# Attention's opening: the second pair's stack half written, half sent, and the first head's score rows in four banks

## The reference

```python
scores = scale * np.matmul(q, k.transpose(0, 1, 3, 2))        # [B, H, 576, 576]
scores = np.where(causal, -1000000000.0, scores)
a = np.exp(scores - scores.max(-1, keepdims=True))
a /= a.sum(-1, keepdims=True) + 1e-09
local = np.matmul(a, v)
q_p = phi(q)                                                   # elu(q) + 1
mem_out = einsum('bhsd,bhde->bhse', q_p, M_prev) / (einsum('bhsd,bhd->bhs', q_p, z_prev)[..., None] + 1e-06)
g = 1 / (1 + exp(-beta))
x = g * mem_out + (1 - g) * local
```

## Time and profile before

| what | value |
|---|---|
| median of 3 runs | 820.97 us |
| the profiled execution | 821.17 us, of which its span 819.4 us |
| TensorE busy | 810.7 us, 99% of the span |
| DVE, ACT, POOL busy | 510.4, 339.6, 339.1 us |
| granted TensorE clock, mean | 0.999 |
| transfers | 49.45 MB |

### The profile page before, as it was taken

How to read it: one execution, slowest core, us unless ns; L and a number is a source line. 1 busy time by engine, 2 the same in 40 slices (tenths; PEclk the granted TensorE clock), 3 DMA queues, 4 the chain that set the end, 5 groups by cost and what they waited for, 6 DMA issues and landing times.

```text
span 819.4 us, 14574 instructions
## 1 busy us (share of the span) xinstructions
PE 810.7 (99%) x5630; PEld 704.2 (86%) x5630; DVE 510.4 (62%) x1052; ACT 339.6 (41%) x608; POOL 339.1 (41%) x453
## 2 busy tenths in 40 slices
PE   8999999999999999999999999999999999999998
PEld 7788888888888888888888899999998888888886
DVE  7877777776588653333433353346688977777762
ACT  6766776675422232222322232233436434333431
POOL 6667676676899930000000000005268844443300
PEclk9999999999999999999999999999999999999999
DMA  8587777866134320000000000000111000000001
GB/s 152 128 178 154 173 167 155 178 142 144 53 103 116 95 73 1 1 1 0 1 1 0 1 1 1 1 1 1 52 51 52 26 27 26 26 14 27 26 14 51
DMA packets 86371, 49.45 MB, mean 60 GB/s; under 512 B 65056, under 2 KB 73248, under 8 KB 86304
## 3 DMA queue, kind: packets, MB, share of 16 engines
q1 hardware_dynamic: 83760, 47.94, 24.3%
q10 hardware_dynamic: 2544, 0.59, 0.4%
HBM read 27.28 MB, written 4.72 MB: 39 GB/s over the span
## 4 chain that ended last, share of the span: by engine, by line
PE 96%; DVE 1%; issue 0%; ACT 0%; POOL 0%; POOLq 0%
PE ps_h L1297 8%; PE ps_y L1313 8%; PE ps_h L1298 8%; PE ps_h L1299 8%; PE ps_y L1314 8%; PE ps_y L1312 8%; PE ps_v L678 5%; PE ps_s L591 4%; PE ps_r L1766 4%; PE ps_r L1764 4%; PE ps_r L1765 4%; PE ps_hid L1701 4%; PE ps_hid L1699 4%; PE ps_hid L1700 3%; PE ps_x L657 3%; PE ps_x L658 3%
## 5 line engine op out<-in xcount | busy, mean ns | idle before, releaser
L1414 DVE TENSOR_TENSOR xT<-xT 128x512 f32<-128x512 f32 (+1 forms) x80 | 61.2, 765 | 127.7 <-ACT xT L1372 127.7
L1598 POOL TENSOR_TENSOR win<-stage,win 128x512 fp32r<-128x512 f32 x2 | 2.6, 1296 | 282.4 <-ACT win L1833 282.4
L1314 PE MATMUL ps_y<-g_hi,wout 128*128 128x512 f32 (+1 forms) x320 | 117.5, 367 | 0.0
L1313 PE MATMUL ps_y<-g_lo,wout 128*128 128x512 f32 (+1 forms) x320 | 117.5, 367 | 0.0
L1312 PE MATMUL ps_y<-g_hi,wout 128*128 128x512 f32 (+1 forms) x320 | 117.4, 367 | 0.0
L1378 ACT ACTIVATE g_hi<-xT 128x512 fp32r<-128x512 f32 (+1 forms) x80 | 47.3, 591 | 135.0 <-DVE xT L1416 135.0
L1297 PE MATMUL ps_h<-x_hi,win 128*128 128x512 f32 (+1 forms) x280 | 103.0, 368 | 0.0
L1299 PE MATMUL ps_h<-x_hi,win 128*128 128x512 f32 (+1 forms) x280 | 102.8, 367 | 0.0
L1298 PE MATMUL ps_h<-x_lo,win 128*128 128x512 f32 (+1 forms) x280 | 102.8, 367 | 0.0
L1372 ACT ACTIVATE xT<-ps_h 128x512 f32<-128x512 f32 (+1 forms) x80 | 44.3, 554 | 139.0 <-PE ps_h L1299 137.2
L1419 DVE TENSOR_TENSOR g_lo<-xT,g_hi 128x512 fp32r<-128x512 f32 (+1 forms) x80 | 65.1, 813 | 52.6 <-ACT g_hi L1378 52.6
(11 more groups left out here) (220 smaller groups left out, 1814.6 us busy)
## 6 DMA issues: line engine op xcount, KB each, us to landing
stacked<-cut SPq DMA_DIRECT2D x56, 288.0 KB, 4.8
out<-res SPq DMA_DIRECT2D x18, 256.0 KB, 2.0
v_raw<-in_v SPq DMA_DIRECT2D x32, 128.0 KB, 2.7
stage<-in_moe_w_in SPq DMA_DIRECT2D x16, 256.0 KB, 2.8
stage<-in_moe_w_out SPq DMA_DIRECT2D x16, 256.0 KB, 2.7
k_raw<-in_k SPq DMA_DIRECT2D x28, 128.0 KB, 2.6
q_raw<-in_q SPq DMA_DIRECT2D x28, 128.0 KB, 3.6
stage<-in_moe_w_in SPq DMA_DIRECT2D x4, 512.0 KB, 3.5
```

What stands on the lines that cost most here:

```text
L1313: pe.matmul(out, wout[:, f, HI, w], g_lo[:, r, 0:n], start=False, stop=False)
L1314: ins = pe.matmul(out, wout[:, f, LO, w], g_hi[:, r, 0:n], start=False, stop=(f == FT - 1))
L1414: dve.tensor_tensor(r, r, r, ALU.mult).then_inc(square_done, 1)
```

## The change

- `DIRECT` goes from 2 to 1: only pair 0 is written in place. Pair 1 is cut like the later ones, but only half of its stack is sent: SP's new `stack(1)` issues two DMAs of 288 KB instead of four, for the halves on the partitions where the parts don't lie already, and ACT writes the other halves with two copies out of `cut` (`third_head`, `fourth_head`: 64 partitions by 2 x 576). SP's order becomes: part of pair 0, keys 1, queries 1, keys 2, queries 2, stack(1), values 0, memory, keys 3, queries 3, values 1, stack(2), keys 4 and on as before.
- Pair 0's six loads are shared: SP issues the first head's key tiles, the half tiles of the keys and the second head's query tiles; ACT the rest. The second pair's loads are all SP's.
- Head 0's score rows: rows 3, 0 and 2 go into the two banks of `ps_x` (`X_AT`), so that TensorE writes all five rows without waiting for a maximum.
- TensorE's order: the second pair's exchanged turns go (ten transposes), its plain turns come after head 0's third rows, head 1's first rows come before head 0's maxima are turned; `WARM` is 8, and two of the `keep_warm` groups go while one changes its place and size.
- POOL: the two doublings go, `repeat_first` for pair 1 goes, `low_queries` is now the first pair's and comes before the first `spread_maxima`, and one memset of 1.5 us comes after it (`fill_others`). ACT: six of the second pair's copies become `round_second_queries`, `round_keys(1)` and the two copies named above; `repeat_queries(1, ...)` is new (two copies). DVE: `low_second_queries` and `cut_keys(1)` take the place of the second pair's four low parts, and `work_out_rest` is moved from after `second_rows(3)` to before `first_rows(2)`.

```diff
 
...
+    DIRECT = 1
+    BY_ACT = ["k_own0", "k_moved0", "q_hi0", "q_cut0", "q_hi1", "q_own1", "third_head", "fourth_head"]
+    BY_DVE = ["k_own1", "k_moved1", "q_lo0"]
+    K_SWAPPED, Q_SWAPPED = 1, 2
...
-    WARM, WARM_BETWEEN = 10, 5
+    WARM, WARM_BETWEEN = 8, 5
...
+    def stack_landed_at(p):
+
+        return 16 * (STACK_DMAS * stacks_sent(p) - (1 if p % SLOTS == 1 else 0))
...
     def cut_is_free(eng, p):
         if p >= DIRECT + 2:
             stacks_taken(eng, p - 2)
-        else:
-            dve_placed(eng, p - 2, "q_lo0")
-
...
+            if p == 3:
+                act_placed(eng, "fourth_head")
+        elif p == 2:
+            dve_placed(eng, "q_lo0")
...
+    def score_rows(h, t):
+
+        if h == 0 and t in X_AT:
+            bank, at = X_AT[t]
+            return ps_x[:, bank, at:at + keys[t]]
+        return ps_s[:, S_AT[t]:S_AT[t] + keys[t]]
...
@@ -304,15 +318,21 @@
             for par in range(2):
                 arrived = stack_landed[p % SLOTS][par]
                 mine, to = words(cut[p % 2][MINE[par], :, :]), slot(2 * p + par)
-                sp.dma_start(words(stacked[0:D, to, :, 0:S]), mine[:, Q_HI:K_HI + 1:2, :]).then_inc(arrived, 16)
-                sp.dma_start(words(stacked[D:P, to, :, 0:S]), mine[:, Q_LO:K_HI + 1, :]).then_inc(arrived, 16)
-
-        load_keys(0)
+                if p > 1 or par == 1:
+                    sp.dma_start(words(stacked[0:D, to, :, 0:S]), mine[:, Q_HI:K_HI + 1:2, :]).then_inc(arrived, 16)
+                if p > 1 or par == 0:
+                    sp.dma_start(words(stacked[D:P, to, :, 0:S]), mine[:, Q_LO:K_HI + 1, :]).then_inc(arrived, 16)
+
+        whole_tiles(sp, first_k, k, 0, 0, k_in[0])
+        half_tiles(sp, first_k, k, 0, k_in[0])
+        whole_tiles(sp, first_q, q, 0, 1, q_in[0])
         load_keys(1)
+        tiles(sp, q_raw[1], q, 1, q_in[1])
         load_keys(2)
         load_queries(2)
+        stack(1)
+        load_values(0)
         load_memory()
-        load_values(0)
         load_keys(3)
         load_queries(3)
         load_values(1)
...
+            pool.wait_ge(cleared, POOL_CLEARS - 1)
+
+        def fill_others():
             pool.memset(words(K1[MINE[0], 1:LATE, 1, 0:S]), 1.0).then_inc(cleared, 1)
             pool.wait_ge(cleared, POOL_CLEARS)
...
+        def repeat_first():
+            act_placed(pool, "q_hi0")
+            pool.tensor_scalar(Q1[MINE[0], 0, 0, 0:S], words(stacked[MINE[0], slot(0), 0, 0:S]), 1.0, 1.0,
                                ALU.mult, ALU.mult).then_inc(repeated, 1)
...
+            act_placed(pool, "q_own1")
+            pool.wait_ge(qT_copied, 1)
+            pool.tensor_tensor(stacked[MINE[1], slot(1), 0, 0:S], qT[0][MINE[1], :], Q1[MINE[1], 0, 1, 0:S],
                                ALU.subtract).then_inc(low_by_pool, 1)
...
-        double(first_k[1], k_in[1])
-        double(first_q[1], q_in[1])
-        pool.wait_ge(doubled_pool, 2)
-        repeat_first(0)
+        repeat_first()
         pool.wait_ge(repeated, 1)
         clear_others()
-        repeat_first(1)
-        pool.wait_ge(repeated, DIRECT)
-        spread_maxima(0)
         low_queries()
         pool.wait_ge(low_by_pool, 1)
+        spread_maxima(0)
+        fill_others()
...
             elif p == 1:
-                act_placed(pe, 0, "k_own0")
+                pe.wait_ge(cleared_dve, DVE_CLEARS + 1)
+                act_placed(pe, "k_own0")
                 pe.wait_ge(k_lo_done, 1)
...
+            rows = score_rows(h, t)
...
+        def turn_maxima(h):
+            need(pe, maxed, 4 * (h + 1))
+            return pe.transpose(ps_s[:, NEG_AT:NEG_AT + P], least[h % 2][:, :], ident[:, :])
...
         def first_rows(h):
             if h == 0:
                 pe.wait_ge(cleared, FOR_ROWS)
...
+                act_placed(pe, "q_hi1")
+                dve_placed(pe, "q_lo0")
+            elif h == 1:
+                act_placed(pe, "q_own1")
+                pe.wait_ge(low_by_pool, 1)
+                pe.wait_ge(maxed, 2)
             elif h < HEADS:
                 p = h // 2
-                pe.wait_ge(stack_landed[p % SLOTS][h % 2], 16 * STACK_DMAS * stacks_sent(p))
-            need(pe, maxed, 4 * min(h, HEADS))
-            if is_head(h - 1):
-                ins = pe.transpose(ps_s[:, NEG_AT:NEG_AT + P], least[(h - 1) % 2][:, :], ident[:, :])
+                pe.wait_ge(stack_landed[p % SLOTS][h % 2], stack_landed_at(p))
+                if p == 1:
+                    act_placed(pe, ("third_head", "fourth_head")[h % 2])
+            if is_head(h - 1) and h != 1:
+                ins = turn_maxima(h - 1)
             if h < HEADS:
                 rows_of_scores(h, 4)
                 ins = rows_of_scores(h, 1)
-            ins.then_inc(scored, 1)
+            if h != 1:
+                ins.then_inc(scored, 1)
...
         def second_rows(h):
-            pe.wait_ge(maxed, 4 * h + 1)
+            need(pe, maxed, 4 * h + 1 if h > 0 else 0)
             rows_of_scores(h, 3).then_inc(scored, 1)
 
         def third_rows(h):
-            pe.wait_ge(maxed, 4 * h + 2)
+            need(pe, maxed, 4 * h + 2 if h > 0 else 0)
             need(pe, neg_done, h)
             rows_of_scores(h, 0)
             rows_of_scores(h, 2).then_inc(scored, 1)
...
             a, p, par = slot(h), h // 2, h % 2
             kept = KEPT[par]
             if h == 0 and c == 0:
-                pe.wait_ge(k_lo_done, 1)
-                act_placed(pe, 1, "q_hi1")
-                dve_placed(pe, 1, "q_lo0")
+                pe.wait_ge(maxed, 4)
                 pe.wait_ge(cleared, FOR_FIRST)
...
             if c == 0:
                 pe.wait_ge(neg_spread, h + 1)
                 if p < DIRECT:
-                    pe.wait_ge(repeated, p + 1)
-                    act_placed(pe, p, "q_own1")
-                    pe.wait_ge(k_lo_done, p + 1)
+                    pe.wait_ge(repeated, 1)
+                    act_placed(pe, "q_own1")
                 else:
...
                 need(pe, t_loc_done, p)
                 if h < 2:
-                    act_placed(pe, 1, "k_own1")
+                    pe.wait_ge(k_hi_done, 1)
                     pe.wait_ge(k_lo_done, 2)
...
         warm_up()
         turn_keys(0)
-        turn_swapped_keys(0)
+        turn_swapped_keys()
         turn_queries(0)
-        turn_swapped_queries(0)
-        act_placed(pe, 0, "k_moved0")
-        dve_placed(pe, 0, "k_moved1")
+        turn_swapped_queries()
+        act_placed(pe, "k_moved0")
+        dve_placed(pe, "k_moved1")
         keep_warm(ps_x[:, 0, 0:P])
         first_rows(0)
-        turn_swapped_keys(1)
-        pe.wait_ge(qT_copied, 1)
-        keep_warm(ps_t[:, 0:P])
         second_rows(0)
+        third_rows(0)
+        turn_queries(1)
         turn_keys(1)
-        turn_queries(1)
-        third_rows(0)
-        turn_swapped_queries(1)
-
         first_rows(1)
-        act_placed(pe, 1, "q_hi1")
-        keep_warm(ps_x[MINE[0], 0, 0:P], 4)
+        turn_maxima(0).then_inc(scored, 1)
+        keep_warm(ps_x[:, 0, 0:P])
+
         cross(0, 0)
         second_rows(1)
         cross(0, 1)
@@ -809,8 +813,9 @@
...
     def scalar(act):
-        tiles(act, first_q[0], q, 0, q_in[0])
-        tiles(act, first_q[1], q, 1, q_in[1])
+        whole_tiles(act, first_k, k, 0, 1, k_in[0])
+        whole_tiles(act, first_q, q, 0, 0, q_in[0])
+        half_tiles(act, first_q, q, 0, q_in[0])
         act.dma_start(beta_in[:, :], beta.unsqueeze(0).broadcast_to([P, H])).then_inc(beta_landed, 16)
...
+            elif what in ("third_head", "fourth_head"):
+                act.wait_ge(k_hi_done, 1)
+                act.wait_ge((q_hi_done, q_lo_done)[what == "fourth_head"], 1)
+                own, to = ((Q_HI, 2), (Q_LO, 3))[what == "fourth_head"]
+                half = MINE[to - 2]
+                place, source = stacked[half, to, :, 0:S], words(cut[1][half, own:K_HI + 1:K_HI - own, :])
...
-        for p, what in BY_ACT:
-            put(p, what)
-            if what == "q_own1":
-                copy_queries(p)
-                if p == 0:
-                    open_gates()
+        def round_second_queries():
+            act.wait_ge(qT_turned, 2)
+            act.activation(cut[1][:, Q_HI, :], ps_t[:, 0:S], ACT.Copy).then_inc(q_hi_done, 1)
+
+        for what in BY_ACT[:-2]:
+            put(what)
+        copy_queries(0)
+        open_gates()
+        round_second_queries()
+        copy_queries(1)
+        round_keys(1)
+        put("third_head")
         exp_weights(0, 0)
         feature_relu(0)
         exp_weights(0, 1)
@@ -903,12 +920,15 @@
         exp_weights(0, 2)
         feature_exp(0)
         exp_weights(0, 3)
+        put("fourth_head")
         round_keys(2)
 
         exp_weights(1, 0)
         feature_relu(1)
         exp_weights(1, 1)
         feature_exp(1)
+        repeat_queries(1, 0)
+        repeat_queries(1, 1)
         exp_weights(1, 2)
         repeat_queries(2, 0)
         exp_weights(1, 3)
...
-            if h == 1:
```

(62 more changed lines are left out.)

120 lines of the change are left out of this document (40 added, 80 removed).

## The result

The changed kernel takes 822.92 us in the median of 12 runs (822.21 to 824.65), the kernel before 821.33 beside it on the same chip (820.72 to 821.90). The ratio is 1.0020, 95% interval 1.0012 to 1.0028. The forecast was 820.8 with a range up to 822.7, so the result lies outside it, on the slow side. The profiled execution took 823.08 us, its span 821.3 [before: 819.4].

The account below looks back on a forecast made before the run. TensorE's lateness in the opening was taken to bound the kernel; the opening's 1.3 us gain, handed back at heads 4 and 6 by the transfer queue, left -0.15: 820.97 - 0.15 = 820.8 us, range 819.0 to 822.7.

Parts of the forecast that it names:

- `z_prev`'s last: Memory loads on SP: issued from about 17.7, the last landing at 24.5, half a microsecond before it is needed.
- the sum for `stack(2)`: SP's queue: half stack at 14.15, two issues 1.3, sixteen loads 12.3, giving 27.8; 27.6 taken, ends 26.5 and 29.1.
- Rival (c): Memory part: z_prev lands at 25.5 instead of 24.5, memory at 25.6, total 820.4; chance 0.07.
- Rival (b): SP's queue binds hard: stack(2) at 29.1, head 6's half 1.35 late, total 822.3, up to 823; chance 0.20.
- The slip: SP's queue: stack(2) 0.6 us late, stack(3) likewise; ends at stack(4), where SP had waited 1.7 us for GpSimd.
- The formula for one transfer: Stack transfers: 288 KB would land 2.7 us after issue, head 6's half at 45.0, and SP's slip would cost nothing.
- Start: Kernel's beginning: keys at 5.1, warm-up ending near 5.2, score rows at 10.0; shift -0.4, ends -0.8 and 0.
- Head 0: Opening: five score rows need no maxima, low second queries end at 14.1, first product at 15.4; shift -2.5.
- Head 1: Opening: work_out_rest takes 1.45 us on VectorE, ending at 19.6; product at 20.8 instead of 22.75, shift -2.0.
- VectorE's low keys: Before the memory part: VectorE's work from 19.6 ends at 24.7, and memory starts at 24.95.
- The opening's sum: Everything gained and kept up to the memory part: 1.3 us, with ends 0.6 and 2.0.
- handed back by the transfer queue: Heads 4 and 6: TensorE waits for late stack halves, so the opening's 1.3 us shrinks to a shift of -0.15.

Follow-up runs that it names:

- e2: Changed kernel with twelve products on the identity filling TensorE's wait before the memory product; 823.65 us, ratio 1.0024 to the kernel before.
- e3: e1 with the four memory loads issued a second time at the changed kernel's place, into an unused strip; 823.94 us, ratio 1.0027 to the kernel before.
- e5: Changed kernel with seven products on the identity filling TensorE's wait before the memory product; 822.36 us, ratio 1.0012 to the kernel before.
- e7: e1 with the first pair's loads not shared, keys on SP and queries on ACT as before; 820.10 us, ratio 0.9988 to the kernel before.
- e8: e1 with head 0's score rows in two banks again; 820.85 us, ratio 0.9993 to the kernel before.
- e6: e1 with GpSimd's last memset moved ahead of the first spreading of maxima; 819.63 us, ratio 0.9980 to the kernel before.
- e1: Changed kernel with the four M_prev and z_prev loads moved ahead of the half stack on SP; 820.17 us, ratio 0.9985 to the kernel before.
- e9: e6 with the second pair's stack sent whole in four DMAs, without ACT's two copies; 825.41 us, ratio 1.0039 to the kernel before.

## Why the prediction was wrong

The forecast started from 820.97; beside the changed kernel the kernel before took 821.33, so 0.36 of the distance is the base. The rest is the change: 0.15 off was forecast, 1.6 on came.

**The step that failed** is the sentence that `z_prev`'s last "landed 6.8 us after the first issue: 24.5, half a microsecond before it is needed". Two terms were too small. The first memory issue came at 18.96, not 17.7: the half stack went out 0.57 later than said (after the late start of this profile; in e2, with an earlier one, it went out at 14.28 and `z_prev` still landed only at 26.2), and 0.7 more came between, where the values' loads were throttled, 2.14 for two instead of 1.15. And from the first issue to the landing it took 8.0 us, not 6.8, because those 6.8 were taken from the kernel before, where no stack transfer stood ahead of them, and here the second `M_prev` issue was itself held for 1.97, where it had taken 1.08. Together 2.5 us late for a slack of 0.5. I had put the throttling behind the stack into the sum for `stack(2)` and left it out of the sum for `z_prev`, which stands in the same queue ahead of it. Rival (c) named this wait and priced it at a landing of 25.5, with a chance of 0.07. Yet this step alone did not lose the forecast: in e3, with `z_prev` early and the queue as late, the stack's wait cost as much.

**What no step priced** is the clock. In the trace a wait of 1.90 us cost 1.90 and 0.9 more. Without it the same late landing would have come out near +0.85 at head 6, as 822.2 or so, by an estimate from that trace (1.75 less 0.9). The changed kernel's own four runs at a mean clock of 1.000 have a median of 822.67. e5, with 822.36, is no direct measurement of it: its memory part starts only 0.21 late, and the rest of its +0.80 comes at heads 4 and 6.

**SP.** The mechanism was right and its size off: `stack(2)` at 29.51, a slip of 2.5 and not 0.6, beyond the 28.5 at which I had called the forecast wrong. Rival (b) had nearly the size (29.1), and its total (822.3 to 823) holds the measured one, but by luck: it priced head 6's wait, and in the changed kernel TensorE waits for no stack. e3 shows that (b)'s wait is real when the memory part is on time, and sooner than I had it, at head 4. The slip ended in front of `stack(4)` as forecast: SP waits there for GpSimd, 1.2 us, and issues it at 55.43. From 45 to 280 us TensorE idles 0.5 us in all, 0.3 more than before.

The formula for one transfer that the prediction quotes from the Trainium skill (DMA: Bandwidth & Descriptors, "Anatomy of one DMA") is given there for transfers issued from GpSimd. These are SP's, so its 2.7 us against 3.3 to 5.3 in the earlier trace rows need not be a matter of load alone; no run here tells.

**Start.** -0.4 was forecast, +0.15 came. The sixteen passes end as said and the transposes start at 5.14, but ten of them ran at the slower rate (1.27 and 1.20 a group, where 0.71 is the later length), and the rows then wait for GpSimd's part. That is within what the start varies by. VectorE's double starts at 5.38 and not 5.1, behind its memset. Sharing the loads moved nothing (e7).

**Head 0.** The five rows need no maxima, as said. First product at 16.14 instead of 15.4: the low second queries end 0.5 later than said, after a start 0.6 later, and 0.3 lies between the end of the spreading (15.82) and the product, where I had allowed 0.1. e8 puts the four banks at 0.7 us.

**Head 1.** I charged `work_out_rest` 1.45 us, half a microsecond net of what had stood in its place; it cost nothing: its three operations take 0.8 us now, and VectorE still waits 0.36 for TensorE behind them. The 1.45 of the earlier trace rows held a wait that I took for work. Its first operation, 0.80 there and 0.18 now, ended with this one on GpSimd:

```profile
30.65 1.42 POOL L397 TENSOR_TENSOR fT<-fT,relu_q 128x576 f32<-128x576 f32 x1
```

The real cost was in `work_out_gates`, where I had none: the memset moved behind the spreading holds its first operation for 1.27 us, of which 0.35 reaches TensorE (e6). The product at 21.45 instead of 20.8.

**VectorE's low keys** end at 25.16 (24.7 said), -0.84 against before; with the memory loads early e1, in a profile whose score rows start 0.44 sooner, keeps -1.27 at memory and -1.17 at head 6, against -1.3 forecast. The opening's sum came out in e1, though its terms are up to 0.3 off (first product 15.70, said 15.4; head 1's 21.01, said 20.8; memory 24.98, said 24.95). The sentence that it is handed back by the transfer queue and by no engine was right too. It was handed back with 1.6 us on top.

The parts of the change, from the experiments: half stack in this order, needed (e9, 5.8 us between the medians against sending it whole); four banks, -0.7 (e8 against e1); shared loads, 0 (e7); the place of the memory loads, +2.8 (the changed kernel against e1; it holds both the wait for `z_prev` and SP's slip); the place of the memset, +0.5 (e1 against e6). The change without the last two is e6.

## What to carry to other kernels

When a step with a wait is put into an in-order queue, compute the landing of every transfer behind it, with the throttled issue times and for the first consumer of each, and not only for the one that bounded the kernel before. Loads that need nothing belong in front of the wait: here four of them cost 2.8 us behind it and nothing ahead. And read the granted clock behind each wait of TensorE's: of waits of some two microseconds the price is not the wait alone.

## What the runs showed of the hardware

- At waits of 1.90 us (changed kernel), 1.89 (e9) and 1.68 (e3) the granted clock fell to 0.50, 0.8 and 0.3 us behind the wait's end in the first two and 0.2 before it in e3, and it stayed there for some 3, 7 and 7 us in which TensorE was busy. Behind waits of up to 1.13 us (e9 at 19.48) it stayed at 1.00. In the profiles of e2 and e5, with products on the identity in the gap, it didn't fall. In four of the changed kernel's twelve runs the mean clock is 1.000, so it doesn't fall so far in every execution.
- TensorE's rate at the start differs between executions of the same code: the second group of five transposes, started at 6.41 and 6.42, took 1.20 us in the changed kernel's profile and 0.76 in e1's, and up to there the two have the same code. The score rows start 0.44 us apart by it (10.58 and 10.14). That this is the clock's rise is an inference from the lengths, which are nearly as far apart as the score-row products' at 0.50 and 1.00 (1.20 and 0.71); the profile shows a granted clock of 1.00 over the whole start.
- A small VectorE operation on SBUF (128x40) takes 0.18 us, and 1.45 beside a GpSimd memset, until that ends. VectorE's low second queries (128x576, a subtraction) beside the same memset kept their 0.76 us (e6, at 13.44).
- Two loads take 1.15 us to issue in a free queue, 2.14 behind two stack transfers of 288 KB, 2.72 behind four. Behind plain loads alone a pair took up to 2.03 (kernel before, at 19.90).
